# Expert layers of a scan–MoE–feed-forward kernel: the hidden tile moved by quarter DMAs and turned on VectorE instead of transposed on TensorE

## What is computed

```python
# 1. a gated complex scan gives x: 3072 tokens x 384
# 2. mixture of 8 experts, one per token
logits = x @ w_gate; e_idx = argmax(logits, axis=1)
gate_w = softmax(logits)[n, e_idx]; eom = sigmoid(x @ w_output_gate)
for e in range(8):
    mask = e_idx == e
    h = maximum(x[mask] @ w1[e], 0.0)          # 384 -> 1024
    out[mask] = gate_w[mask] * eom[mask, e] * (h @ w2[e])   # 1024 -> 384
# 3. feed-forward on all tokens
h = out @ w_in; g = maximum(0.01 * h, h); y = g @ w_out     # 384 -> 2048 -> 384
```

## Time and profile before

| | |
|---|---|
| median of 3 runs | 981.19 us |
| the profiled execution's own time | 978.09 us |
| its span, first to last instruction | 976.3 us |
| TensorE busy (matmul) | 940.3 us, 96% |
| VectorE, ScalarE, GpSimd busy | 438.7, 441.9, 510.1 us |
| mean granted TensorE clock | 0.996 of full speed |
| expert stage on TensorE, first `layer1` to first `ff1` | 298.0 to 569.1 us |

### The profile page before, as it was taken

The page is one execution under the profiler, slowest core; times in us unless marked ns, Lnnn a source line. Parts: engine busy times, 40 slices in busy tenths (PEclk is TensorE's granted clock), DMA queues, the critical chain, the costliest instruction groups (busy, mean ns, idle before and its releaser), DMA issues.

```text
span 976.3 us, 18188 instructions
## 1 busy us (share of the span) xinstructions
PE 940.3 (96%) x5904; PEld 836.7 (86%) x5905; DVE 438.7 (45%) x794; ACT 441.9 (45%) x742; POOL 510.1 (52%) x429
## 2 busy tenths in 40 slices
PE   5999999999879999999999999999999999999997
PEld 4777878887877989989999898999998999999997
DVE  5898898898846333433433432222222122222111
ACT  7999888997711222222222333333333333333322
POOL 4134656656464986767759923343243433423433
PEclk9999999999989999999999999999999999999999
DMA  3642363340153645335355520010010000000000
GB/s 121 205 139 83 113 238 99 101 137 2 64 183 94 205 133 167 113 105 169 113 169 169 130 57 17 9 41 17 9 49 17 29 21 17 33 1 1 33 1 32
DMA packets 74123, 83.89 MB, mean 86 GB/s; under 512 B 57653, under 2 KB 63305, under 8 KB 71497
## 3 DMA queue, kind: packets, MB, share of 16 engines
q1 hardware_dynamic: 67048, 47.20, 17.5%
q0 software_dynamic: 6144, 34.65, 10.2%
q10 hardware_dynamic: 864, 1.19, 0.3%
HBM read 65.59 MB, written 17.38 MB: 85 GB/s over the span
## 4 chain that ended last, share of the span: by engine, by line
PE 77%; ACT 10%; DVE 5%; issue 5%; DMA 1%; POOL 1%; ACTq 1%; SPq 0%; POOLq 0%; DVEq 0%
PE bank L2168 21%; PE bank L2181 20%; PE bank L2156 12%; PE bank L2131 12%; PE bank L2141 3%; PE bank L1098 2%; DVE neglog L850 1%; PE bank L1180 1%; PE bank L1138 1%; PE bank L1166 1%; PE bank L1140 1%; PE bank L1108 1%; PE bank L1121 1%; DVE neglog L857 1%; ACT log_sq L643 1%
## 5 line engine op out<-in xcount | busy, mean ns | idle before, releaser
L1922 POOL TENSOR_TENSOR act_r<-act_f,act_r 128x512 fp32r<-128x512 f32 x96 | 124.7, 1298 | 258.2 <-ACT act_r L1984 258.1
L2181 PE MATMUL bank<-w_out_r,act_r 128*128 128x384 f32 x1152 | 216.6, 336 | 0.3 <-POOL act_r L1922 0.3
L2168 PE MATMUL bank<-x,w_in_r 128*128 128x512 f32 x864 | 215.7, 394 | 0.0
L2181 PEld LDWEIGHTS bank<-w_out_r,act_r 128*128 128x128 f32 x1152 | 203.8, 188 | 9.1 <-POOL act_r L1922 0.6
L2063 DVE TENSOR_TENSOR act_f<-bank,small 128x512 f32<-128x512 f32 x96 | 66.5, 692 | 286.9 <-ACT small L1981 286.9
L2168 PEld LDWEIGHTS bank<-x,w_in_r 128*128 128x128 f32 x864 | 160.6, 187 | 30.1
L1981 ACT ACTIVATE small<-bank 128x512 f32<-128x512 f32 x96 | 57.5, 599 | 194.7 <-PE bank L2168 194.5
L2131 PE MATMUL bank<-wm,x_tr 128*128 (+1 forms) x522 | 129.1, 401 | 1.5 <-issue 1.0
L2156 PE MATMUL bank<-wm,h_tr 128*128 (+1 forms) x696 | 125.6, 336 | 0.0
L2156 PEld LDWEIGHTS bank<-wm,h_tr 128*128 128x128 f32 x696 | 121.5, 188 | 2.5
L2131 PEld LDWEIGHTS bank<-wm,x_tr 128*128 128x128 f32 x522 | 96.0, 188 | 23.3 <-issue 2.2
(11 more groups left out here) (195 smaller groups left out, 1363.9 us busy)
## 6 DMA issues: line engine op xcount, KB each, us to landing
stage<-moe_w POOLq DMA_DIRECT2D x12, 1536.0 KB, 7.3
qkv_in<-in_qkv SPq DMA_DIRECT2D x24, 576.0 KB, 6.0
a_in<-in_a SPq DMA_DIRECT2D x11, 768.0 KB, 5.2
stage<-moe_w SPq DMA_DIRECT2D x4, 1536.0 KB, 7.1
x_q<-x_sorted SPq DMA_DIRECT2D x116, 48.0 KB, 1.9
y_sorted<-y_b SPq DMA_DIRECT2D x29, 192.0 KB, 1.9
xg<-y_sorted SPq DMA_DIRECT2D x96, 48.0 KB, 1.9
stage<-w_out POOLq DMA_DIRECT2D x2, 1536.0 KB, 7.0
```

The lines of the kernel that those rows point to most:

```text
L1922: pool.tensor_tensor(a[:, 1, :], act_f[f % 2][:, :], a[:, 0, :].bitcast(F32), ALU.subtract).then_inc(s_gl, 1)
L2168: last = pe.matmul(h_bank[f % 2][:, :], w_in_r[:, wp, t * F2 + f * P:t * F2 + (f + 1) * P], window_part(w, xp)[:, t, :], start=(t == 0 and ...
L2181: last = pe.matmul(o_bank[j][:, 0:W], a[:, ap, j * P:(j + 1) * P], w_out_r[:, wp, f * W:(f + 1) * W], start=(f == 0 and n == 0), stop=(f = ...
```

## The change

`transpose_hidden` is gone. In its place `h` is moved within SBUF to a new tile `h_q` by sixteen DMAs a block, each 32 partitions x 256 columns (32 rows of 1 KB), eight issued by SyncE and eight by ScalarE; VectorE then turns `h_q` in squares into banks 2 and 3 by two instructions (`turn_hidden`). `w2`'s rows are laid out by quarters on the host to match. `layer2` runs two blocks behind `layer1` instead of one. `leading` waits for the halves of `layer2` of the block before. At the end, the first two `ff1` go before the last `layer2`, and the tokens of the feed-forward stage have two buffers `xg` instead of four.

```diff
+    def move_quarter(eng, a, done):
+        n = F1 // Q
+        for b in range(Q):
+            eng.dma_start(h_q[a * SQ:(a + 1) * SQ, b * n:(b + 1) * n],
+                          h[b * SQ:(b + 1) * SQ, a * n:(a + 1) * n]).then_inc(done, 16)
 # SyncE
+        def hidden_quarters(g):
+            sp.wait_ge(s_h, 2 * g + 2)
+            need(sp, s_hth, 2 * g)
+            for i in range(2):
+                move_quarter(sp, 2 * i + 1, s_hq[1])
-        with sp.Fori(1, third) as g:
-            load(g + 3)
-            gates(g + 2)
+        with sp.Fori(1, early) as g:
+            load(g + 4)
+            hidden_quarters(g + 2)
+            gates(g + 3)
             store(g)
...
         for t in range(2):
             tile_in(t)
-        gates(third + 2)
+        hidden_quarters(early + 2)
+        gates(early + 3)
+        store(early)
         for t in range(2, TW):
             tile_in(t)
+        hidden_quarters(early + 3)
 # ScalarE
         def relu(g):
             act.wait_ge(s_gate_in, 16 * g + 16)
+            for i in range(2):
+                need(act, s_hq[i], 128 * g)
             act.wait_ge(s_p1, g + 1)
...
+        def hidden_quarters(g):
+            need(act, s_hth, 2 * g)
+            act.wait_ge(s_h, 2 * g + 2)
+            for i in range(2):
+                move_quarter(act, 2 * i, s_hq[0])
-        with act.Fori(0, third + 1) as g:
+        with act.Fori(1, early + 1) as g:
             leading(g)
-            relu(g + 1)
-        leading(third + 1)
+            relu(g + 2)
+            hidden_quarters(g + 2)
+        leading(early + 1)
         for j in range(2):
             tokens(0, j)
-        relu(third + 2)
+        relu(early + 3)
+        hidden_quarters(early + 3)
         for j in range(2, TW):
             tokens(0, j)
-        leading(third + 2, third + 2)
+        leading(early + 2)
+        leading(early + 3)
 # VectorE
+        def turn_hidden(g):
+            for i in range(2):
+                dve.wait_ge(s_hq[i], 128 * g + 128)
+            need(dve, s_hl, 2 * g)
+            for j in range(2):
+                dve.transpose(th_bank[j][:, :].rearrange("p (k b i) -> p b k i", b=Q, i=SQ),
+                              h_q[:, :].rearrange("p (b k j) -> p b k j", b=Q, j=SQ)[:, :, 4 * j:4 * j + 4, :]
+                              ).then_inc(s_hth, 1)
-        with dve.Fori(1, third + 1) as g:
+        with dve.Fori(1, early + 1) as g:
             trailing(g)
-            turn_tokens(g + 2)
-            block_tokens(g + 2)
+            turn_tokens(g + 3)
+            turn_hidden(g + 1)
+            block_tokens(g + 3)
             result(g)
 # TensorE
-        transpose_hidden(0)
         layer1(1)
+        layer1(2)
         layer2(0)
-        with pe.Fori(1, third + 1) as g:
-            transpose_hidden(g)
-            layer1(g + 1)
+        with pe.Fori(1, early + 2) as g:
+            layer1(g + 2)
             layer2(g)
...
+        layer2(early + 2)
         pe.wait_ge(s_wh, 2 * (E + 2))
         ff1(0, 0)
-        pe.wait_ge(s_y, third + 3)
         ff1(0, 1)
+        layer2(early + 3)
```

More of the change, by code:

```diff
@@ L1735, in experts_then_feed_forward @@
     h = sb(ctx, "h", [P, F1])
+    h_q = sb(ctx, "h_q", [P, F1])
     h_tr = sb(ctx, "h_tr", [P, 2, F1], F32R)
@@ L1741, in experts_then_feed_forward @@
     o_sb = [late(f"o_sb{i}", [P, W]) for i in range(TW)]
-    xg = [sb(ctx, f"xg{i}", [P, W]) for i in range(TW)]
+    xg = [sb(ctx, f"xg{i}", [P, W]) for i in range(2)]
     x2 = [sb(ctx, "x2_0", [P, 2, KT, XW], F32R),
@@ L1756, in experts_then_feed_forward @@
     s_h = sem("hidden_ready")
+    s_hq = [sem(f"hidden_quarters{i}_in") for i in range(2)]
     s_hth = sem("hidden_transposed")
@@ L1762, in experts_then_feed_forward @@
     s_ys = sem("block_stored")
-    s_in = [sem(f"tokens{i}_in") for i in range(TW)]
+    s_in = [sem(f"tokens{i}_in") for i in range(2)]
     s_tt = sem("tokens_transposed")
@@ L1847, in layers_sync @@
         load(2)
+        hidden_quarters(0)
         gates(1)
+        load(3)
+        hidden_quarters(1)
+        gates(2)
         sp.wait_ge(s_table, 1)
-        third = second_before_last(sp)
-        load(3)
-        gates(2)
+        early = third_before_last(sp)
+        load(4)
+        hidden_quarters(2)
+        gates(3)
         store(0)
-        with sp.Fori(1, third) as g:
-            load(g + 3)
-            gates(g + 2)
+        with sp.Fori(1, early) as g:
+            load(g + 4)
+            hidden_quarters(g + 2)
+            gates(g + 3)
             store(g)
@@ L1863, in layers_sync @@
             tile_in(t)
-        gates(third + 2)
+        hidden_quarters(early + 2)
+        gates(early + 3)
+        store(early)
         for t in range(2, TW):
             tile_in(t)
[L1867 to L1870, removed]
+        hidden_quarters(early + 3)
+        store(early + 1)
+        store(early + 2)
+        store(early + 3)
+        sp.wait_ge(s_ys, early * 16 + 64)
         for t in range(TW, 2 * TW):
@@ L1954, in relu, with leading @@
                                scale=gate_b[:, 0:1]).then_inc(s_h, 1)
-        def leading(g, late=None):
-            act.wait_ge(s_hth, g + 1)
+        def hidden_quarters(g):
[3 more added lines that the diff above has]
+                move_quarter(act, 2 * i, s_hq[0])
+        def leading(g):
             for j in range(2):
-                if j == 1 and late is not None:
-                    act.wait_ge(s_p2, late)
+                need(act, (s_half, s_p2)[j], g)
+                act.wait_ge(s_hth, 2 * g + j + 1)
                 act.activation(h_tr[:, 0, j * 512:(j + 1) * 512], th_bank[j][:, :], ACT.Copy).then_inc(s_hh, 1)
@@ L2034, in block_tokens, with trailing @@
                               ALU.subtract).then_inc(s_xl, 1)
-        def trailing(g, parts=(0, 1)):
-            for j in parts:
+        def trailing(g):
+            for j in range(2):
                 half = slice(j * 512, (j + 1) * 512)
@@ L2100, in layers_vector @@
             tokens(0, j + 1)
[L2101 to L2104, removed]
+            if j == 0:
+                turn_hidden(early + 2)
+        result(early + 1)
+        trailing(early + 2)
+        turn_hidden(early + 3)
+        result(early + 2)
+        trailing(early + 3)
+        result(early + 3)
         for f in range(2):
@@ L2134, in layer1, with layer2 @@
             last.then_inc(s_p1, 1)
[L2136 to L2145, removed]
+        def layer2(g):
             base = weights_of(g, 2)
             wmf = wm[:, :, :, :].rearrange("p s l n -> p (s l n)")
-            if to_bank is ye_bank:
-                need(pe, s_y, g)
+            need(pe, s_y, g)
             for t in range(FT1):
-                if t == FT1 // 2 and amid is not None:
-                    transpose_hidden(amid)
                 if t % 4 == 0:
```

81 lines of the change are left out of this document (43 added, 38 removed).

## The result

The changed kernel takes **1083.45 us** (median of 4 runs, 1079.49 to 1091.58) beside 980.82 us before (median of 4, 977.83 to 982.62): ratio 1.106, 95% interval 1.0989 to 1.1131. It is slower, as forecast, but by 102.6 us and not by 27; the range ended at 1027. The profiled execution is the slowest of the four, 1091.58 us.

A forecast was written before the change was run, and what follows sets the result against it. TensorE bound the kernel, and SyncE's queue was to take over the loop. Start 7, loop 6.5, end 7 and late landings 6 gave +26.5 on 978.1, 1004.6; with 3.1 for the median, 1008 us, range 976 to 1027.

The forecast's parts named there:

- SyncE becomes the bound of the loop: Expert loop: SyncE's work rises to 9.5 us a block, over TensorE's 8.38 and the present 9.25; +6.5 us over 26 rounds.
- I take 0.47: SyncE's queue: each quarter DMA costs 0.47 us with its gap, eight a block 3.8 us.
- the high end of the bounds: SyncE's queue: dearest price considered for a quarter's issue, 0.56 us with the gap, from `carry`, the one DMA within SBUF.
- Late landings: Expert loop: quarters landing late behind 1.5 MB weight transfers hold up `layer1`; +6 us, from 0 to 15.
- Start +7: Start of the expert stage: third `layer1` and `layer2(0)` wait behind the quarters' issues, gate column and `leading(0)`; +7 us.
- end +7: After the loop: `layer2(27)` waits for tile DMAs, quarters, gate column and `leading(27)`, TensorE idle some 7.6 us; +7 us.
- GpSimd's weights: Split of `w_in` on GpSimd, 51.5 us: hidden with SyncE as bound; at full speed `ff1` would wait 5 us.
- VectorE and ScalarE: Expert loop: VectorE 5.2 us of 8.4, ScalarE 6.2 plus loop code, under 8.38; neither a bound by itself.
- Transposes −25.2: TensorE in the expert loop: eight transposes a block removed, 0.87 us over 29 blocks, −25.2 us of its time.
- rival 2: Expert loop: issues are no bound at all, 8.38 us a block, −11 us, 970 us; chance 0.06.
- Rival 3: SyncE's queue: a copy within SBUF issues like `carry`, 0.56 us; 10.1 to 10.2 a block, +47, 1028 us; chance 0.15.
- rival 1: SyncE's queue: issues are cheap, 0.37 us, and the loop gains 14; in all 0 to −4 us; chance 0.14.

The follow-up runs named there:

- order alone: The changed kernel's new order of work, but with the hidden tile transposed on TensorE as before and no quarter DMAs: 995.64 us, ratio 1.0153.
- light version of the change: The changed kernel with the twelve weight transfers of experts 2 to 7 cut from 1.5 MB to 32 KB: 1061.62 us, ratio 1.0817.
- issues alone: Order alone plus eight constant 32 x 256 copies within SBUF a block on SyncE, awaited only by the next eight: 1038.06 us, ratio 1.0579.
- light version through DRAM: The version through DRAM with the weight transfers of experts 2 to 7 cut from 1.5 MB to 32 KB: 981.65 us, ratio 1.0029.
- version through DRAM: The changed kernel with `h` written to DRAM by one DMA and read back by four, all on ScalarE, `turn_hidden` behind `block_tokens`: 1023.94 us, ratio 1.0417.

## Why the prediction was wrong

Right were the sign, the engine named ("SyncE becomes the bound of the loop"), and that TensorE's saved 0.87 us would turn into idle time. Medians of the runs put 102.3 us together (order alone is taken against 981.16, the kernel before beside it):

| | us |
|---|---|
| order alone, against before | +14.5 |
| eight issues a block on SyncE, against order alone | +42.4 |
| weight transfers, the change against its light version | +21.8 |
| the rest, light version of the change against issues alone | +23.6 |

The last row is a difference of two unlike runs: the light version has copies that depend on `h`, ScalarE's eight too, and no large transfers, the run with issues alone has them and the transposes. It is no price of one thing.

Step by step:

1. **"I take 0.47, the row nearest in what I think matters, fixed addresses in a row."** This is the step that failed. A copy within SBUF costs the queue 0.648 us in the mean (the median issue is 0.591), of 1, 2 or 4 KB a row. The nearest row was `carry`, the only one within SBUF. Even that gives 0.56, so the high end of the bounds was too low. SyncE's work is 10.9 us with the issues alone, so 25 rounds take 42 us more than before and not 6.5 more; the price alone is 8 x (0.648 − 0.47) x 25 = 36 of the 76 us by which the forecast was short. That fixed addresses matter isn't borne out. In the scan stage of the kernel before, loads from DRAM with fixed addresses take 0.58 us to issue, more than any row that the bounds were taken from:

```profile
L408 SPq DMA_DIRECT2D qkv_in<-in_qkv x24: 334/582/1581, 2.9 to 214.8; - x24
```

   Nor does the place of the data alone set the price: from DRAM there are 0.33 (`load`), 0.43 (`xg`) and 0.58 here. What sets it stayed open.
2. **Late landings, +6, at most 15.** Measured 21.8 for all that the weight transfers cost, some 17 without the longer issues, above the bound. The bound counted ten delays of 1.5 us and let the rest be caught up. But a queue with no slack catches little up: SyncE waited 23.4 of 310 us and worked the rest. The step had the mechanism and too small a size.
3. **The rest.** It had no term. Between issues alone and light weights the loop takes 0.6 us a block more (11.535 against 10.94), 15 us: 0.1 are waits, 0.1 eight issues of 0.661 in place of 0.648, the other 0.4 are spread over the gaps of the queue and weren't settled. The other 9 us lie at the start and the end, where the run with issues alone has no copies.
4. **Start +7, end +7.** Measured +9.9 and +16.2. At the start the third `layer1` came when forecast (322.30 less the scan stage's 5.4, beside 316.8); then it ran 6.19 us in place of 4.2, and ScalarE's copies held `leading(0)` longer. In the end's chain most of the excess is the copies: eight issues of SyncE from 653.68 to 658.65, then eight of ScalarE from 662.85 to 667.86, 10 us where the forecast had 3.9 + 3.8 (in between the gate column, 1.9 us from issue to `relu`); the eight tile reads ahead of them take 4.9, not 3.8. TensorE idles 11.06 us before `layer2(27)` (forecast some 7.6), and that pass runs 6.09 us in place of 4.17. Idle times of 2.14 us before `layer2(26)` and 1.41 behind `layer2(28)` had no term.
5. **GpSimd's weights.** Rightly hidden: in the change the split ends at 653.9 us, and the first `ff1` starts at 676.6. With the order alone it ends later too, and `ff1` still doesn't wait for it. "At full speed `ff1` would wait 5 us" was never met: at the 8.7 us a block of the light version through DRAM the end's chain runs through tile reads and `leading(27)`.
6. **VectorE and ScalarE.** A turn takes 701 ns (780 by size), and VectorE is no bound. ScalarE's eight issues take 5.0 us, not 3.8. `leading` stands behind them (148.1 us of waits between 320 and 650 us), but nothing shows it as the bound of the loop: SyncE's queue is on the chain. No run has the copies on one queue only with `h` waiting for them, so ScalarE's share isn't measured.
7. **Transposes −25.2.** The size is right where the loop runs freely: 8.4 us a block.
8. **The rivals and sums.** The rule of rival 2 (the Trainium skill, "DMA: Bandwidth & Descriptors", section "Issuing engines are not separate DMA queues", the issue is "usually small relative to the DMA itself") is true of one copy, 0.6 us beside a landing of some 2, and decides nothing here: the queue pays eight a block. Rival 3 was the nearest, at 0.56 us and 1028. Two sums of the prediction don't come out: rival 1 with landings of 2 to 6 is −14 + 12 + 2 to 6, so 0 to +4 and not "0 to −4", and the forecast's own 20.5 us with landings of 0 to 10 is 1002 to 1012, not 999. Neither changes the verdict.

## What to carry to other kernels

Before work is moved from a compute engine to DMAs, add up a block's issues on the queue that takes them, and compare the sum with the period. Take the price from the most similar DMA in the trace, and set the high end of the bounds above the dearest: here it was 0.65 us within SBUF, and issues of one queue ran from 0.31 to 0.61 in the medians. If the queue becomes full and waits for landings itself, it catches little of a late one up, and an order that runs further ahead costs fill and drain that the loop must first earn. A wait at the top of the list is no cause by itself: moving the gate column changed its name, not the time. Nor is a releaser's name: where several semaphores are waited for, look at what the engine's own queue did in that time.

## What the runs showed of the hardware

- A copy of 32 rows within SBUF takes 0.59 us to issue whether its rows are 1, 2 or 4 KB. Four reads from DRAM that regroup 128 pieces of 1 KB each take 1.77 us with the address code between them, 0.44 each, and a write of 512 KB takes 0.39.
- Small DMAs issued within some microseconds of a 1.5 MB transfer land after 6 to 8 us in place of 1.8. Six transfers of 2 KB rows in its place leave the time of the version through DRAM the same (ratio 1.0407 beside 1.0417).
- After idle stretches of 2 to 5 us passes often ran partly at a granted clock of 0.50, such as the `layer1` of 7.27 us in place of 4.21. Holding the clock up with extra transposes brought nothing.
